# Step 0 of a linear-attention kernel: weight copies and masks move from GpSimd to ScalarE and VectorE, queries load later

## The reference

```
k_n = k / (norm(k) + 1e-6)
for t in range(S):
    y[t] = q[t] @ state
    state = state + beta[t] * outer(k_n[t], v[t] - k_n[t] @ state)
```

## Time and profile before

| | |
|---|---|
| time, median of 3 runs | 1094.85 us (1093.78 to 1095.8) |
| the profiled execution's own time | 1094.22 us |
| its span, first to last instruction | 1092.4 us |
| TensorE busy | 1046.3 us, 96% of the span |
| VectorE busy | 589.8 us, 54% |
| ScalarE busy | 409.9 us, 38% |
| GpSimd busy | 30.1 us, 3% |
| chain of waits, share by engine | TensorE 81%, VectorE 15%, issue 2%, ScalarE 1% |
| mean granted TensorE clock | 0.984 of full |

### The profile page before, as it was taken

How to read it: one execution, slowest core, us unless ns; L and a number is a source line. 1 busy time by engine, 2 the same in 40 slices (tenths; PEclk the granted TensorE clock), 3 DMA queues, 4 the chain that set the end, 5 groups by cost and what they waited for, 6 DMA issues and landing times.

```text
span 1092.4 us, 24184 instructions
## 1 busy us (share of the span) xinstructions
PE 1046.3 (96%) x10828; PEld 850.5 (78%) x10828; DVE 589.8 (54%) x977; ACT 409.9 (38%) x669; POOL 30.1 (3%) x33
## 2 busy tenths in 40 slices
PE   6768899999999999999999999999999999999996
PEld 4356677777777777777787888888888888888885
DVE  6958957947948876892356534324324333333222
ACT  3322354454354355344466644232232232222211
POOL 5300000000000000000000000000000000000000
PEclk9968999999999999999999999999999999999999
DMA  9413101400410230040021211110200200100101
GB/s 254 127 32 88 30 3 36 113 3 2 115 33 2 60 88 3 4 144 2 3 87 58 87 49 68 33 26 1 59 1 1 58 1 1 30 1 1 30 1 29
DMA packets 19031, 48.05 MB, mean 44 GB/s; under 512 B 2448, under 2 KB 9232, under 8 KB 17872
## 3 DMA queue, kind: packets, MB, share of 16 engines
q1 hardware_dynamic: 18928, 46.51, 15.7%
HBM read 37.06 MB, written 9.44 MB: 43 GB/s over the span
## 4 chain that ended last, share of the span: by engine, by line
PE 81%; DVE 15%; issue 2%; ACT 1%; POOL 0%; DVEq 0%; POOLq 0%; ACTq 0%
PE bank L671 21%; PE acc L1234 15%; PE hps L1219 14%; PE acc L690 10%; PE hps L671 7%; DVE outer L986 4%; DVE inv L990 4%; PE hps L690 4%; DVE g L1051 1%; PE bank L1179 1%; PE bank L1165 1%; PE bank L1143 1%; DVE g1l L1058 1%; PE bank L1132 1%; PE bank L1121 1%
## 5 line engine op out<-in xcount | busy, mean ns | idle before, releaser
L588 ACT ACTIVATE g<-bank 128x512 f32<-128x512 f32 x72 | 43.1, 598 | 257.4 <-PE bank L671 142.7
L1219 PE MATMUL hps<-xh,w1h 128*128 128x512 f32 x288 | 120.9, 420 | 5.1 <-DVE g L1051 4.8
L1234 PE MATMUL acc<-g1h,w2h 128*128 128x512 f32 x288 | 119.6, 415 | 2.2 <-DVE g1l L1058 2.1
L893 ACT ACTIVATE g1h<-g 128x512 fp32r<-128x512 f32 x96 | 60.7, 632 | 155.5 <-DVE g L1051 139.5
L1219 PE MATMUL hps<-xh,w1l 128*128 128x512 f32 x288 | 113.9, 395 | 0.0
L1234 PE MATMUL acc<-g1h,w2l 128*128 128x512 f32 x288 | 113.8, 395 | 0.0
L1219 PE MATMUL hps<-xl,w1h 128*128 128x512 f32 x288 | 113.8, 395 | 0.0
L1234 PE MATMUL acc<-g1l,w2h 128*128 128x512 f32 x288 | 113.7, 395 | 0.0
L1058 DVE TENSOR_TENSOR g1l<-g,g1h 128x512 fp32r<-128x512 f32 x96 | 66.2, 689 | 68.0 <-ACT g1h L893 67.6
L1051 DVE SCALAR_TENSOR_TENSOR g<-hps,g 128x512 f32<-128x512 f32 x96 | 65.7, 685 | 61.3 <-ACT g L887 61.0
L884 ACT ACTIVATE g<-hps,half_c 128x512 f32<-128x512 f32 x96 | 65.6, 683 | 61.6 <-PE hps L1219 61.6
(11 more groups left out here) (192 smaller groups left out, 2041.0 us busy)
## 6 DMA issues: line engine op xcount, KB each, us to landing
kqT<-kq SPq DMA_DIRECT2D x22, 384.0 KB, 6.3
v_in<-v SPq DMA_DIRECT2D x6, 768.0 KB, 4.3
k_in<-k SPq DMA_DIRECT2D x6, 768.0 KB, 5.4
x2d<-x2s SPq DMA_DIRECT2D x18, 256.0 KB, 5.6
x2t<-x2d SPq DMA_DIRECT2D x6, 768.0 KB, 6.4
y<-y_t SPq DMA_DIRECT2D x48, 96.0 KB, 2.2
stage<-w_in SPq DMA_DIRECT2D x4, 768.0 KB, 10.2
stage<-w_out SPq DMA_DIRECT2D x4, 768.0 KB, 9.7
```

The source lines that it names most:

```text
L893: act.activation(g1h[:, f % 2, :], g1[:, f % 2, :], ACT.Copy).then_inc(s_gh, 1)
L1219: last = pe.matmul(hps[f % 2][:, :], wt[:, kk, P * f:P * f + P], xx[:, kk, :], start=(kk == 0 and e == 0), stop=(kk == KD - 1 and e == 2))
L1234: last = pe.matmul(acc[j][:, :], wt[:, f, P * j:P * j + P], gg[:, f % 2, :], start=(f == 0 and e == 0), stop=(f == NF1 - 1 and e == 2))
```

## The change

The weight copies ("hi") go to ScalarE, two chunks ahead of their pieces in the list; the first stands before the norm's square root, the second behind it. The scaling of step 0's v goes to VectorE in two halves ("vnh"). ScalarE no longer copies step 0's query products out: VectorE masks them straight from PSUM (the second half in an event of its own, "GQE"). The query products move from the front of step 0 to behind X and behind KU of the first half. Of the pieces, 20 instead of 22 stand beside the inversion, two right behind it and ahead of Z, and the last two behind the first query product and behind U. The order of U, KU, PU, KS, QS, the half transposes and XE behind is rewritten, the last KU standing behind XE, and the banks with it. The sync queue loads step 0's queries, k and step 1's keys behind the sixth weight chunk instead of before the fifth. In the code:

```diff
@@ -92,10 +92,11 @@
...
 NPIECE = NCHUNK * PIECES
-BESIDE = 22
+BESIDE = 20
 
...
 def first_body():
+
 
...
@@ -104,35 +105,38 @@
...
         for p in pieces[:n]:
-            ev += ([("hi", 0, p // PIECES)] if p % PIECES == 0 else []) + [("piece", 0, p)]
+            ev.append(("piece", 0, p))
             if p >= 2:
                 ev.append(("low", 0, p - 2))
+            if p % PIECES == 0 and p // PIECES + 2 < NCHUNK:
+                ev.append(("hi", 0, p // PIECES + 2))
         del pieces[:n]
...
             break
+        if e[0] == "nrm":
+            out.append(("hi", 0, 0))
         out.append(e)
-        if e[0] == "sys":
-            out += [("GQ", 0, hf) for hf in range(HALVES)]
+        if e[0] == "nrm":
+            out.append(("hi", 0, 1))
         if e[0] == "inv":
             out += split(BESIDE * (e[2] + 1) // INV - BESIDE * e[2] // INV)
-            if e[2] == 10:
-                out += [("mask", 0, n) for n in range(NQ)]
-            if e[2] == 20:
-                out += [("vn", 0, 0)] + [("GK", 1, hf) for hf in range(HALVES)]
+            if e[2] == 21:
+                out += [("GK", 1, hf) for hf in range(HALVES)]
 
...
 
-    out += [("ft", 0, 0), ("Z", 0, 0), ("Z", 0, 1), ("xd", 0, 0)] + split(2)
-    out += [("X", 0, 0), ("X", 0, 1), ("low", 0, NPIECE - 2), ("low", 0, NPIECE - 1), ("ft", 0, 1), ("ft", 0, 2)]
-    out += [("U", 0, 0)] + turn(0) + [("KU", 0, 0), ("PU", 0, 0)] + turn(1) + [("KS", 0, 1), ("QS", 0, 1)] + turn(2) + [("U", 0, 1)]
-    out += turn(3) + [("PU", 0, 1)] + turn(4) + [("KU", 0, 1)] + turn(5)
-    assert not pieces
-    out += [(kind, 0, n) for kind in ("XT", "XE") for n in range(KD)]
+    out += split(2) + [("low", 0, NPIECE - 4), ("low", 0, NPIECE - 3)]
+    out += [("ft", 0, 0), ("Z", 0, 0), ("Z", 0, 1), ("xd", 0, 0), ("X", 0, 0), ("X", 0, 1), ("ft", 0, 1), ("ft", 0, 2), ("vnh", 0, 0)]
+    out += [("GQ", 0, 0), ("piece", 0, NPIECE - 2), ("low", 0, NPIECE - 2), ("U", 0, 0), ("piece", 0, NPIECE - 1)] + turn(0)
+    out += [("low", 0, NPIECE - 1), ("KU", 0, 0), ("vnh", 0, 1)]
+    out += [("GQ", 0, 1), ("KS", 0, 1), ("GQE", 0, 1), ("PU", 0, 0), ("U", 0, 1), ("QS", 0, 1)] + turn(1)
+    out += [("PU", 0, 1)] + turn(2) + turn(3)
+    out += [(kind, 0, n) for kind in ("XT", "XE") for n in range(KD)] + [("KU", 0, 1)] + turn(4) + turn(5)
     return out, [e for e in inversion(1) if e[0][0] != "tr"]
...
@@ -198,10 +202,10 @@
...
 NPSUM = NBANK + 2 + KD
-FIRST = {("GK", 0, 0): (0, 1), ("GK", 0, 1): (3, 4), ("GQ", 0, 0): (2, 0), ("GQ", 0, 1): (1, 3), ("GK", 1, 0): (3, 4), ("GK", 1, 1): (0, 1),
-         ("Z", 0, 0): (2,), ("Z", 0, 1): (3,), ("X", 0, 0): (4,), ("X", 0, 1): (0,), ("U", 0, 0): (1, 2), ("KU", 0, 0): (5, 6),
-         ("PU", 0, 0): (3, 4), ("KS", 0, 1): (0, 7), ("QS", 0, 1): (1, 2), ("U", 0, 1): (5, 6), ("KU", 0, 1): (5, 6),
-         ("XT", 0, 0): (0,), ("XT", 0, 1): (7,), ("XT", 0, 2): (4,)}
+FIRST = {("GK", 0, 0): (0, 1), ("GK", 0, 1): (3, 4), ("GK", 1, 0): (3, 4), ("GK", 1, 1): (0, 1),
+         ("Z", 0, 0): (0,), ("Z", 0, 1): (3,), ("X", 0, 0): (4,), ("X", 0, 1): (2,), ("GQ", 0, 0): (1, 0), ("U", 0, 0): (3, 4),
+         ("KU", 0, 0): (0, 1), ("GQ", 0, 1): (2, 3), ("KS", 0, 1): (4, 5), ("PU", 0, 0): (6, 7), ("U", 0, 1): (0, 1),
+         ("QS", 0, 1): (4, 5), ("KU", 0, 1): (2, 7), ("XT", 0, 0): (0,), ("XT", 0, 1): (1,), ("XT", 0, 2): (6,)}
 
...
@@ -420,7 +424,7 @@
...
             s_const0, s_const, s_neg = sem("const_zeroed"), sem("const_ready"), sem("negative_ready")
-            s_zero, s_raw = sem("inverse_zeroed"), sem("prob_copied")
+            s_zero = sem("inverse_zeroed")
             s_wh, s_wp, s_wl = sem("w_hi_ready"), sem("w_lo_summed"), sem("w_lo_ready")
...
@@ -736,13 +740,15 @@
...
                     sp.wait_ge(s_kq[0][0], 16 * BP)
-                    load_kq(0, (1,))
                     for n in range(NSTAGE):
...
                     load_v(0)
+                    load_w(NSTAGE)
+                    load_w(NSTAGE + 1)
+                    load_kq(1, (0,))
+                    load_kq(0, (1,))
                     load_k(0)
-                    load_kq(1, (0,))
-                    for n in range(NSTAGE, NCHUNK):
+                    for n in range(NSTAGE + 2, NCHUNK):
                         load_w(n)
...
@@ -803,19 +809,6 @@
...
                     pool.wait_ge(s_const, N_CONST)
-                    for kind, c, n in PLANS[0]:
-                        if kind == "mask":
-                            pool.wait_ge(s_raw, n + 1)
-                            pool.tensor_tensor(prob[:, H * n:H * n + H, :], prob[:, H * n:H * n + H, :],
-                                               later[:, :].unsqueeze(1).to_broadcast([P, H, C]), ALU.mult).then_inc(s_gq, 1)
-                        elif kind == "hi":
-                            pool.wait_ge(s_w[n % NSTAGE], 16 * (n // NSTAGE + 1))
-                            pool.tensor_copy(w_chunk(w1h, w2h, n), stage_as(n)).then_inc(s_wh, 1)
-                        elif kind == "vn":
-                            pool.wait_ge(s_v, 16)
-                            pool.wait_ge(s_n, N_NRM)
-                            pool.tensor_tensor(v_in[:, :, :], v_in[:, :, :], ntok[:, :].unsqueeze(2).to_broadcast([P, NINST, D]),
-                                               ALU.mult).then_inc(s_vn, 1)
                     for c in range(1, NSTEP):
...
@@ -833,12 +826,6 @@
...
                                     .then_inc(s_gk, NQH // own)
-                        elif kind == "GQ" and c == 0:
-                            act.wait_ge(p_gq, half(c, hf))
-                            for j in range(NQH):
-                                q = NQH * hf + j
-                                act.activation(prob[:, H * q:H * q + H, :],
-                                               bank_of(u, j)[:, :].rearrange("p (i t) -> p i t", t=C), ACT.Copy).then_inc(s_raw, 1)
                         elif kind == "nrm":
...
@@ -902,7 +889,11 @@
...
                         kind, _, p = u
-                        if kind == "low":
+                        if kind == "hi":
+                            n = p
+                            act.wait_ge(s_w[n % NSTAGE], 16 * (n // NSTAGE + 1))
+                            act.activation(w_chunk(w1h, w2h, n), stage_as(n), ACT.Copy).then_inc(s_wh, 1)
+                        elif kind == "low":
                             act.wait_ge(s_wp, p + 1)
...
@@ -1002,7 +993,13 @@
...
                                 .then_inc(s_ft, 1)
-                        elif kind == "vn" and c:
+                        elif kind == "vnh":
+                            dve.wait_ge(s_v, 16)
+                            dve.wait_ge(s_n, N_NRM)
+                            part = slice(NPAIR * q, NPAIR * q + NPAIR)
+                            dve.tensor_tensor(v_in[:, part, :], v_in[:, part, :],
+                                              ntok[:, part].unsqueeze(2).to_broadcast([P, NPAIR, D]), ALU.mult).then_inc(s_vn, 1)
+                        elif kind == "vn":
                             dve.wait_ge(s_v, 16 * (c + 1))
...
@@ -1018,8 +1015,8 @@
...
                                             bank_of(out_of(c, q), 1)[:, 0:BIG]).then_inc(s_y2, 1)
-                        elif kind == "GQ" and c:
-                            hf = q
+                        elif (kind, c, q) == ("GQE", 0, 1) or kind == "GQ" and (c, q) != (0, 1):
+                            hf, u = q, ("GQ", c, q)
                             dve.wait_ge(p_gq, half(c, hf))
...
@@ -1028,7 +1025,7 @@
...
                             dve.wait_ge(p_ks, half(c, hf) - 1)
-                            dve.wait_ge(s_vn, c + 1)
+                            dve.wait_ge(s_vn, c + HALVES)
                             for j in range(NQH):
...
@@ -1081,7 +1078,7 @@
...
                                 else:
-                                    pe.wait_ge(s_raw if v[:2] == ("GQ", 0) else evicted[v[0]], evictions(v, j))
+                                    pe.wait_ge(evicted[v[0]], evictions(v, j))
 
...
```

## The result

| | before | after |
|---|---|---|
| median of 17 runs | 1094.9 us (1092.07 to 1096.2) | 1097.33 us (1096.23 to 1099.23) |
| the profiled execution | 1094.22 us | 1098.84 us (span 1097.0) |
| step 1's first norm operation starts | 92.50 | 96.96 |
| TensorE's first product of Z starts | 60.03 | 62.67 |

The ratio is 1.0026, with a 95% interval of 1.0019 to 1.0034: the change makes the kernel slower by 2.4 us (difference of the medians), where I had forecast 3 us faster. The profiled execution of after lies 1.5 us above its median; differences between single traces are read with that in mind.

What follows compares the result with a forecast made beforehand. VectorE until Z, then TensorE, ScalarE and VectorE by turns bound step 0. Z 3.2 us later plus a 26.1 us stretch instead of 32.5 ends step 0 3.0 us earlier: 1094.85 - 3.0 = 1091.8 us, range 1084 to 1102.

Steps and rivals of the forecast that it cites:

- GpSimd beside VectorE: Step 0's inversion on VectorE: without GpSimd's work it ends 15.5 us earlier, at 42.5, but loads hide the gain.
- The copies in ScalarE's order, and the queue: Ahead of Z: copies wait in series for loads, load 6 queues until 47.9, Z starts at 63.2 instead of 60.03.
- The low clock back near 58.5: TensorE's pieces ahead of Z: half clock after idling from 41 to 50, nearly full again after 8 us of work.
- the slower rival: Behind Z: granted clock falls again, twelve products and two pieces lose 10.6 us, time 1102.4; chance 0.25.
- From Z to the end of step 0: 26.1 us: Z to step 1's first norm operation: 26.1 us instead of 32.5, with products at 1.1 us, ending step 0 at 89.5.
- the 1.9 us stop: TensorE's stall inside PU behind Z: assumed to stay, raising the stretch from 24.2 to 26.1 us.
- 16.4 us from Z to the end of PU: Behind Z: products and pieces 9.8 us, state's update 1.1, KS 1.1, then PU, U, QS, PU 4.4.
- The new order: Behind Z: query products moved there, each priced at 1.1 us, filling waits for ScalarE's evictions or lying beside VectorE's work.
- The sum: Whole kernel: median 1094.85 less 3.0 us, so 1091.8 us expected.

Runs made afterwards that it cites:

- the two last ones: Changed kernel with weights 6 and 7 first, copies one chunk ahead, step 1's queries early: 1083.44 us; same with query products ahead of Z, loads reordered: 1080.33 us.
- the repeated product: Changed kernel with step 1's queries loaded early (1097.32 us), plus step 0's second query product computed five times instead of once: 1104.12 us, ratio 1.0084.

## Why the prediction was wrong

- **GpSimd beside VectorE.** Right: 31 pairs in 21.25 us (forecast 21.2), first transpose at 42.62 (42.5). Putting the copies back costs 7.1 us there.
- **The copies in ScalarE's order, and the queue.** Right, each copy within 0.7 us, Z within 0.6, and the cause is shown three ways: loading the weights first, putting the copies one chunk ahead, and GpSimd's own order bring Z forward by 6.8, 9.8 and 10.8 us.
- **The low clock back near 58.5.** It was full from 56. The clock did fall again behind Z (0.77 and 0.71 in 72 to 88), as the slower rival had it, but it is the smaller part of the loss: with a clock of 0.95 the stretch still took 32.4 us of after's 34.3. A product at half clock (1.92 us) takes little more than the packets allow anyway, 1.75. The rival's price of 10.6 us came true nowhere.
- **From Z to the end of step 0: 26.1 us. This step failed, and in one term.** I priced each product of 64 small matmuls at the 1.1 us of the earlier trace rows, and kept the 1.9 us stop of the earlier trace rows as a single one that "nothing says" goes. That row is of step 1, where large matmuls of the first network stand around a product. Behind Z there are, but for two pieces, only small ones, and they come at 3.5 us per 127, 1.75 us a product. I had 16.4 us from Z to the end of PU; in the run with the copies one ahead it was 24.4 (52.99 to 77.4). By the packets' pace the 13 products (832 matmuls) make 22.9, and the low clock around 61 us some 1.4 (from Z to KU's first matmul 11.4 us there, 10.0 in after, where it was full). The rest, from v's copy to the norm, was forecast as 7.8 and took 7.9 there.
- **The new order.** I took the move of the query products behind Z as free but for their 1.1 us. It is 128 matmuls moved from a stretch in which TensorE idles for 9 us to the one in which instructions are scarce: 3.5 us, by the run with the products back (1097.33 to 1093.81) and, less directly, by the two last ones (1083.44 to 1080.33). With them back, nothing is left of what the change loses against before.
- **The sum.** 1097.33 against 1091.8 is 5.5 us; the stretch behind Z was 8.2 us longer than forecast in a trace 1.5 us above its median, with Z 0.5 us early. That leaves 6.2 against 5.5, which I take for scatter between single traces.

What I should have read: the 1.90 us of the earlier trace rows stood in the middle of a product of 64 at a place where nothing was awaited, and the window from 68 to 76 of the earlier trace rows had 262 small matmuls in 8 us at a clock of 0.93, 2 us for 64. A part of those 8 us is ScalarE's evictions (TensorE was busy 4.8), so the row gives no clean price, but a row of the very stretch was at hand, and I priced by one from elsewhere.

## What to carry to other kernels

Price an instruction by a row from the stretch in which it will stand: a burst of tiny matmuls can be bound by how fast its instructions arrive, and an idle stretch ahead of it is the place to move some of them to. Idle time put down to "issue", and repeated at even spacing, points to a rate and not to an accident. And when an engine that waits for loads also does the work that releases the next load, each load's latency comes in series; put the releasing work ahead of the waiting copy in the order.

## What the runs showed of the hardware

TensorE's instructions arrived as 16 KB packets, about 127 small matmuls with their weight loads, 3.4 to 3.9 us apart where it had used up what it held, and each stop by "issue" ended 2.3 to 3.1 us behind the start of such a packet. Two transfers of 384 KB in flight at that time went with a gap of 7 us between packets and a stop of 2.53 us instead of about 1. That it is this fetch that TensorE waits for is read from the spacing, the count and the packets' times, and borne out by the repeated product; no run changed the fetch itself. VectorE's operations on two inputs took 1.2 to 2.9 us beside GpSimd's copies, masks and scaling, and 0.2 to 0.4 without.
